# One load moved ahead of another in the start-up, and the elementwise work of the last layer (scaled halves of the token shift, low parts of the squares, splits of w_r and w_v) spread anew over ScalarE, VectorE and GpSimd

## The reference, cut to what matters

```python
x = attention(q, k, v, i_gate, f_gate, o_gate)     # (2, 768, 320)
# MoE1: gated layer that mixes over the tokens
h = relu(x @ w_in); u, v = h[..., :512], h[..., 512:]
v_n = (v - mean(v)) / sqrt(var(v) + 1e-6)
v_s = einsum('ts,bsd->btd', w_spatial, v_n) + b_spatial
y = (u * v_s) @ w_out                               # (2, 768, 320)
# MoE2: token shift, squared relu, sigmoid gate
y_prev = y shifted by one token (0 at the first)
xk = mu_k * y + (1 - mu_k) * y_prev
xr = mu_r * y + (1 - mu_r) * y_prev
k = relu(xk @ w_k)                                  # (2, 768, 1024)
out = sigmoid(xr @ w_r) * ((k * k) @ w_v)
```

## Time and profile before

| what | value |
|---|---|
| median of 3 runs | 332.5 us (332.32 to 332.51) |
| the profiled execution's own time | 331.42 us |
| its span in the trace | 329.70 us |
| TensorE busy | 311.5 us (94%) |
| VectorE busy | 213.9 us (65%) |
| ScalarE busy | 140.7 us (43%) |
| GpSimd busy | 69.2 us (21%) |
| mean granted TensorE clock | 0.978 of full |

### The profile page before, as it was taken

The page is one execution under the profiler, slowest core; times in us unless marked ns, Lnnn a source line. Parts: engine busy times, 40 slices in busy tenths (PEclk is TensorE's granted clock), DMA queues, the critical chain, the costliest instruction groups (busy, mean ns, idle before and its releaser), DMA issues.

```text
span 329.7 us, 5470 instructions
## 1 busy us (share of the span) xinstructions
PE 311.5 (94%) x1952; PEld 297.8 (90%) x1952; DVE 213.9 (65%) x458; ACT 140.7 (43%) x271; POOL 69.2 (21%) x94
## 2 busy tenths in 40 slices
PE   7899889999999999678999999999799999999996
PEld 3798789999999999579999999999699999999996
DVE  7788798767567747653642689979489536845111
ACT  4945574333332332550313354367584255336000
POOL 8622413012212100511111120214041013013000
PEclk9989879999999999999999999999799999999999
DMA  5994122022234207200006002040000100010011
GB/s 155 272 226 120 56 82 73 22 71 84 84 98 127 75 4 231 88 0 3 0 2 191 0 2 61 2 159 0 2 0 7 56 1 2 20 40 2 20 51 50
DMA packets 11374, 20.92 MB, mean 63 GB/s; under 512 B 1908, under 2 KB 5508, under 8 KB 11348
## 3 DMA queue, kind: packets, MB, share of 16 engines
q1 hardware_dynamic: 11348, 20.58, 21.1%
HBM read 18.53 MB, written 1.97 MB: 62 GB/s over the span
## 4 chain that ended last, share of the span: by engine, by line
PE 73%; DVE 14%; issue 4%; ACT 4%; DMA 3%; SPq 1%; POOL 1%; DVEq 0%; ACTq 0%; POOLq 0%
PE ps_v L1079 17%; PE ps_s L1079 10%; PE ps_e L1079 7%; PE ps_in L1079 6%; PE ps_out L1079 6%; PE ps_t L1079 6%; PE ps_in L1157 4%; PE ps_z L1079 4%; PE ps_s L1148 4%; DMA qkt<-in_qk 3%; PE ps_out L1167 2%; PE ps_z L1176 2%; DVE kr L1051 1%; PE ps_e L1125 1%; DVE pt L804 1%
## 5 line engine op out<-in xcount | busy, mean ns | idle before, releaser
L539 POOL TENSOR_TENSOR kkl<-kr,kkh 128x384 fp32r<-128x384 f32 x16 | 17.6, 1097 | 73.4 <-ACT kkh L694 73.4
L1051 DVE TENSOR_TENSOR kr<-kr 128x384 f32<-128x384 f32 x32 | 20.4, 641 | 14.5 <-ACT kr L737 14.5
L1148 PEld LDWEIGHTS ps_s<-qkt 128*128 128x128 f32 x192 | 25.9, 200 | 3.6 <-DMA qkt<-in_qk 2.0
L1148 PE MATMUL ps_s<-qkt 128*128 128x128 f32 x192 | 27.1, 287 | 1.7 <-DMA qkt<-in_qk 1.7
L1157 PEld LDWEIGHTS ps_in<-tok,pt 128*128 128x128 f32 x192 | 24.6, 195 | 0.9
L1157 PE MATMUL ps_in<-tok,pt 128*128 128x42 f32 x192 | 24.4, 278 | 0.0
L1079 PE MATMUL ps_v<-win,xth 128*128 128x512 f32 x60 | 21.9, 431 | 1.3 <-DVE xtl L885 1.3
L710 ACT ACTIVATE gh<-ut 128x384 fp32r<-128x384 f32 x16 | 8.4, 525 | 33.4 <-DVE ut L1016 33.3
L574 ACT ACTIVATE et<-ps_e 128x512 f32<-128x512 f32 x24 | 14.3, 595 | 18.8 <-PE ps_e L1130 14.4
L534 POOL TENSOR_TENSOR gl<-ut,gh 128x384 fp32r<-128x384 f32 x8 | 9.5, 1183 | 58.5 <-ACT gh L710 58.5
L1079 PE MATMUL ps_v<-xth,win 128*128 128x384 f32 x65 | 19.1, 359 | 2.5 <-ACT vr L580 1.4
(11 more groups left out here) (293 smaller groups left out, 917.1 us busy)
## 6 DMA issues: line engine op xcount, KB each, us to landing
tok<-in_vk SPq DMA_DIRECT2D x12, 328.0 KB, 4.3
qkt<-in_qk SPq DMA_DIRECT2D x24, 160.0 KB
sp_raw<-in_w_sp SPq DMA_DIRECT2D x6, 384.0 KB, 5.0
osig<-in_og SPq DMA_DIRECT2D x2, 960.0 KB, 10.5
out_y<-ob SPq DMA_DIRECT2D x12, 160.0 KB, 1.8
wv_raw<-in_w_v SPq DMA_DIRECT2D x2, 640.0 KB, 4.9
win_raw<-in_w_in SPq DMA_DIRECT2D x4, 256.0 KB, 7.0
wk_raw<-in_w_k SPq DMA_DIRECT2D x2, 512.0 KB, 4.5
```

Of the source, the lines that this page charges most:

```text
L539: gp.tensor_tensor(kkl[a % 2][:, b, :], kr[n % 4][:, :], bits(kkh[a % 2][:, b, :]), ALU.subtract).then_inc(sems["kk_lo_pool"], 1)
L1051: ve.tensor_tensor(kr[n % 4][:, :], kr[n % 4][:, :], kr[n % 4][:, :], ALU.mult).then_inc(sems["kk_done"], 1)
L1148: last = te.matmul(ps_s[j][:, h * CH:(h + 1) * CH], keys[u % NS][:, HH * j + h, :], queries[u % NS][:, h, :], start=True, stop=True)
```

## The change

It has five parts. (1) SyncE issues the features of the third chunk before the first half of w_in. (2) The `scaled` half of each shift step goes from VectorE to ScalarE: step 0 of a block behind the swap of y, step n+1 behind the same group as `shifted_hi` of step n, ahead of it. (3) All low parts of the squares are made on VectorE. (4) w_r is split earlier: ScalarE and VectorE behind sp(3,1), ScalarE behind sp(3,2), and the two full low blocks by GpSimd behind sp(3,2). (5) w_v is split by ScalarE behind k(0,3) to k(0,6), with a wait for its load, and by VectorE behind r(0,2) and the three groups of y(2). The load of w_v stays where it was.

```diff
+WV_LO = {("r", 0, 2): (0,), ("y", 2, TA): (1,), ("y", 2, TB): (2,), ("y", 2, TL): (3,)}
...
@@ SyncE
             load_tokens(1)
+            load_features(2)
             load_win(0)
-            load_features(2)
             load_win(1)
...
@@ GpSimd, in the loop over GROUPS
-                if kind == "k" and b % 2 == 0:
-                    n = 8 * a + b
-                    pool.wait_ge(sems["kk_hi_done"], n + 1)
-                    gp.tensor_tensor(kkl[a % 2][:, b, :], kr[n % 4][:, :], bits(kkh[a % 2][:, b, :]),
-                                     ALU.subtract).then_inc(sems["kk_lo_pool"], 1)
+                if key == ("sp", 3, 2):
+                    for t in range(2):
+                        pool.wait_ge(sems["wr_hi"], 2 + t)
+                        gp.tensor_tensor(wr[:, 2 + t, :], wr_raw[:, t, :], bits(wr[:, t, :]),
+                                         ALU.subtract).then_inc(sems["wr_lo"], 1)
...
@@ ScalarE
+            def scale(a, n):
+                t, w = n // 2, n % 2
+                i = 6 * a + n
+                if i == 0:
+                    act.wait_ge(sems["mu_in"], 16)
+                act.wait_ge(sems["y_copied"], 2 * a + 2)
+                if t == TL:
+                    act.wait_ge(sems["y_left"], a + 1)
+                if i > 1:
+                    act.wait_ge(sems["x_shifted"], i - 1)
+                sc.activation(scaled[:, n % 2, :], yt[a % 2][:, t, 1:NB + 1], ACT.Copy,
+                              scale=mucol[:, w, t:t + 1]).then_inc(sems["x_scaled"], 1)
...
+                    if (a, b) == (3, 1):
+                        left_hi(wr, wr_raw, "wr_in", 64, "wr_left", "wr_hi")
+                    if (a, b) == (3, 2):
+                        rows_hi(wr, wr_raw, "wr_left_lo", "wr_hi")
...
                     sc.activation(ysw[64:128, :], ps[0:64, 0:NB], ACT.Copy).then_inc(sems["y_swapped"], 1)
+                    scale(a, 0)
                 if kind == "k":
                     n = 8 * a + b
-                    if n == 0:
-                        left_hi(wr, wr_raw, "wr_in", 64, "wr_left", "wr_hi")
-                        rows_hi(wr, wr_raw, "wr_left_lo", "wr_hi")
                     act.wait_ge(sems["group_mm"], p + 1)
                     if n >= 4:
-                        act.wait_ge(sems["kk_lo_pool"], (n - 4) // 2 + 1)
-                        act.wait_ge(sems["kk_lo_dve"], (n - 4 + 1) // 2)
+                        act.wait_ge(sems["kk_lo_dve"], n - 3)
...
-                    if a == 1 and 1 <= b <= 4:
-                        f = 2 * (b - 1)
+                    if a == 0 and 3 <= b <= 6:
+                        f = 2 * (b - 3)
                         act.wait_ge(sems["wv_in"], 32)
+                        act.wait_ge(sems["g_lo_pool"], 2 * NBLK)
+                        act.wait_ge(sems["g_lo_dve"], 2 * NBLK)
                         sc.activation(wv_hi[:, f:f + 2, :], wv_raw[f // 4][:, f % 4:f % 4 + 2, :],
...
                 for i in SHIFTS.get(key, ()):
+                    if i % 6 < 5:
+                        scale(i // 6, i % 6 + 1)
                     shifted_hi(i // 6, i % 6)
...
@@ VectorE, shift()
-                if i > 1:
-                    dve.wait_ge(sems["x_shifted"], i - 1)
-                ve.tensor_scalar(scaled[:, n % 2, :], y[:, t, 1:NB + 1], mucol[:, w, t:t + 1], None,
-                                 ALU.mult).then_inc(sems["x_scaled"], 1)
                 dve.wait_ge(sems["x_scaled"], i + 1)
...
+                    if (a, b) == (3, 1):
+                        left_lo(wr, wr_raw, "wr_left", "wr_left_lo")
...
-                    if n == 0:
-                        left_lo(wr, wr_raw, "wr_left", "wr_left_lo")
-                        rows_lo(wr, wr_raw, "wr_hi", "wr_lo")
...
-                    if b in (2, 4, 6):
+                    if b > 0:
                         square_lo(n - 1)
                     if b == 7:
                         square_lo(n)
-                    if a == 1 and 2 <= b <= 5:
-                        f = 2 * (b - 2)
-                        dve.wait_ge(sems["wv_hi_done"], b - 1)
...
+                for i in WV_LO.get(key, ()):
+                    f = 2 * i
+                    dve.wait_ge(sems["wv_hi_done"], i + 1)
+                    ve.tensor_tensor(wv_lo[f // 4][:, f % 4:f % 4 + 2, :], wv_raw[f // 4][:, f % 4:f % 4 + 2, :],
+                                     bits(wv_hi[:, f:f + 2, :]), ALU.subtract).then_inc(sems["wv_lo_done"], 1)
...
@@ TensorE, before the first v group of a block
-                        pe.wait_ge(sems["kk_lo_pool"], 4 * a + 4)
-                        pe.wait_ge(sems["kk_lo_dve"], 4 * a + 4)
+                        pe.wait_ge(sems["kk_lo_dve"], 8 * a + 8)
```

More of the change, by code:

```diff
@@ L147 @@
 gate_m gate_next gates_in group_mm gwt_done head_rows_done ident_done ident_zero later_done later_zero ones_done k_relu
-kk_done kk_hi_done kk_lo_dve kk_lo_pool kw_done kw_zero mix_biased mix_gated mrow_in
+kk_done kk_hi_done kk_lo_dve kw_done kw_zero mix_biased mix_gated mrow_in
 mu_done mu_in nm_hi_done nm_zero nm_lo_done num_done o_in0 o_in1 osig_done out_done0 out_done1 out_ready
@@ L1056, in _ @@
                         square_lo(n)
-                    if a == 1 and 2 <= b <= 5:
-                        f = 2 * (b - 2)
-                        dve.wait_ge(sems["wv_hi_done"], b - 1)
-                        ve.tensor_tensor(wv_lo[f // 4][:, f % 4:f % 4 + 2, :], wv_raw[f // 4][:, f % 4:f % 4 + 2, :],
-                                         bits(wv_hi[:, f:f + 2, :]), ALU.subtract).then_inc(sems["wv_lo_done"], 1)
+                for i in WV_LO.get(key, ()):
[3 more added lines that the diff above has]
+                                     bits(wv_hi[:, f:f + 2, :]), ALU.subtract).then_inc(sems["wv_lo_done"], 1)
                 if kind == "v":
```

## The result

| | median | lowest to highest | runs |
|---|---|---|---|
| kernel before, run beside it | 332.5 us | 332.32 to 333.99 | 4 |
| changed kernel | 329.51 us | 327.85 to 330.02 | 4 |

The medians differ by 3.0 us; the forecast was 329.6. The ratio of the two kernels is 0.9892 (95% interval 0.9846 to 0.9938).

The account below looks back on a forecast made before the run. TensorE bounded the kernel, losing 4.17 us to its wait for VectorE at k(1,0) and the half clock behind it. Gains of 1.2 (wait) and 1.7 (clock), 2.9 together, took 332.5 to 329.6; range 328.0 to 332.0.

Parts of the forecast that it names:

- The sum: Whole kernel: 1.2 us less wait at k(1,0), 1.7 from the clock, 0 from the rest, 2.9 less in all.
- The path through w_v's load: ScalarE in k(0) waits 0.8 for w_v, step 11 completes at 232.0, the wait at k(1,0) shrinks from 2.49 to 1.3.
- the slower rival: w_v's load holds ScalarE and delays step 11 one for one; landing at 224 gives 333.9 us; chance 0.12.
- The table load: Before the first sigmoid: 1.28 by the trace; the skill's further drain of 1.38 would leave the wait at k(1,0) unshrunk.
- The scaled half on the path: Step 11's scaled copy on ScalarE, between first sigmoid and `shifted`: taken at 0.53 us, bounds 0.41 to 0.73.
- The clock: Behind k(1,0): a stall of 1.3 us keeps the full clock, another 1.7 gained; rival that it falls, chance 0.17.
- The prediction's second leg: TensorE's 2.0 us stall for `sp_lo` kept the clock at 1.00, so the shorter stall of 1.3 should too.
- Features first: Start-up: w_in's first half lands at about 21.2, harmless up to 21.8; value nothing, at worst a loss of 0.5 us.
- The first relu "because nothing stands between": Head of k(0): with w_r's pieces gone, the first relu comes at about 217.5 instead of 219.76.
- The load of w_v "where it was": End of sp(3): last product with u unmoved, so w_v's load is issued at 215.37 and lands at 221.4.
- The cause named: In sp(3,3), GpSimd's two low parts of w_r, 0.85 us each, can hold up VectorE, returning its saving on scaled halves.
- The squares' low parts: In k(0), moving them from GpSimd to VectorE is even for VectorE, from nothing to 0.5 us better.

Follow-up runs that it names:

- E8: Changed kernel with three more ScalarE copies, computing nothing new, ahead of the first sigmoid: median 332.93 us, ratio 1.0018.
- E3: Changed kernel with shift steps 10 and 11 behind k(0,0) and k(0,1) instead of r(0,0) and r(0,1): median 326.86 us, ratio 0.9878.
- E6: Changed kernel with the split of w_v put back in k(1): median 328.04 us, ratio 0.9873.
- E7: Changed kernel with the split of w_r put back at the head of k(0): median 327.9 us, ratio 0.9862.
- E5: Changed kernel with the scaled halves back on VectorE: median 335.09 us, ratio 1.0065.
- E9: Kernel before with only the scaled halves moved to ScalarE: median 326.75 us, ratio 0.9847.
- E1: Kernel before with only the third chunk's features issued ahead of w_in's first half: median 331.84 us, ratio 1.0013.
- E2: Changed kernel with w_in's first half issued ahead of the third chunk's features again: median 329.24 us, ratio 0.9933.
- E4: Changed kernel with the low parts of the even squares back on GpSimd: median 329.41 us, ratio 0.9937.
- E11: Kernel before with only the squares' low parts all made on VectorE: median 328.79 us, ratio 0.9888.
- E12: Changed kernel with w_r's two full low blocks moved from GpSimd in sp(3) to VectorE at the head of k(0): median 328.74 us, ratio 0.9892.
- E10: Kernel before with scaled halves on ScalarE and all the squares' low parts on VectorE: median 328.14 us, ratio 0.9878.

## Why the prediction was right, and where its terms were not

**The sum.** Predicted 2.9, made of 1.2 of wait and 1.7 of clock. Measured from S on 1.18 and 1.63, and 3.0 between the medians. That the median met the forecast to 0.1 is luck: the interval of the ratio is 0.46% wide to each side, 1.5 us, where the prediction had thought that 0.2% could be told. The two sections of the profile, 2.81 together, are the better witness.

**The path through w_v's load** is right. ScalarE's wait 1.00 (0.8 predicted), table load 17.05 behind S (17.24 predicted: 227.95 less 210.71), wait at k(1,0) 1.31 (1.3). From the first piece of w_v to the table load it was 6.55, as summed up. Behind the table load it was 4.30 and not 4.08, mostly since `shifted` began 0.29 behind the end of the scaled half (231.41 to 231.70) and not 0.03; the table load's being 0.19 sooner made up for it. E8 shows that nothing of the path is slack, E3 that all of the wait goes when step 11 leaves it, E6 and E7 that it goes, or shrinks to 0.37, when w_v's pieces leave ScalarE or the load comes in time. "One for one" with the landing, as the slower rival had it, was not tested by itself: in E5 the first relu was late too.

**The table load.** The sigmoid started 1.29 behind the start of the load again (229.17 to 230.46). The further drain of 1.38 that the Trainium skill counts (ScalarE: Activation LUTs, What ACT_TABLE_LOAD costs) isn't seen here either; by it, as an estimate, the wait would have been 2.7.

**The scaled half on the path** was taken at 0.53 and took 0.61, inside its bounds. Each of the 24 costs ScalarE more than VectorE, as the Trainium skill says of operations with a fast mode on VectorE (Perfetto Trace Analysis, Optimizing Scalar/DVE Operations), and the trace agrees (0.61 against 0.41). The page names a saturated VectorE as the case in which moving such work may make sense; it doesn't say "only", as the prediction has it. VectorE's 65% of the whole span would have misled here: up to the end of sp(3) VectorE was the engine that set the first relu and w_v's load, and E9, this part alone, gave the best ratio of all.

**The clock.** Kept, as predicted. Behind k(1,0), waits of 2.3 to 3.8 in the lists (before, E1, E5, E8) all dropped it, and waits of 0.2 to 1.1 (changed, E2, E4, E7, E11, E12) never did. Nothing between was measured there. The prediction's second leg, that a stall of 2.0 keeps it, was one execution's luck: see the end.

**Features first.** Nothing, as predicted: w_in's first half landed near 20.8 (21.2 in E1), predicted 21.2, under the 21.8 from which it would cost.

**Two terms were credited to the wrong part,** and their errors cancelled.

- *The first relu "because nothing stands between".* It did come 2.8 earlier (6.26 behind S for 9.05; predicted 217.5, 6.79). But not from w_r's pieces: without moving them it is 6.35 (E7) and 6.36 (E9). It comes from the scaled halves, for which the prediction had allowed 0.45 at step 9, with the rest given back to GpSimd's pieces. They save 2.69 there, 1.38 of it before sp(3) began, where the prediction had looked for nothing. w_r's pieces give 1.88 at the head of k(0) (from step 9's high part to the first relu 0.43, and 2.31 in E9) and take 1.78 in sp(3) (step 9's high part 5.83 behind S in the changed kernel, 4.05 in E9). E5 agrees: w_r moved without the scaled halves makes the first relu no sooner than before, but later (9.67 for 9.05).
- *The load of w_v "where it was".* It was, to 0.46 (4.20 for 4.66), because part 4 gave back 1.79 of the 2.24 that part 2 gained (E9: 2.42). E7 shows the price: 0.94 of wait. The cause named was GpSimd; E12 shows that it is VectorE's stand for ScalarE, and less than 0.1 of GpSimd.

**The squares' low parts,** "for VectorE this is even, from nothing to 0.5 better", turned out otherwise where nothing hides them: they shorten relu to table load by 1.16 (E11). The prediction had priced every collision by the one square of 1.10, which is 0.56 dearer than one of 0.54; two of the three that count cost 0.8. It had priced a low part at 0.55, and one behind the other they come every 0.47. In the changed kernel the prediction came out right all the same, since ScalarE's wait for w_v hides it (E4).

**What the whole could have been.** In steps, by the wait at k(1,0): before 2.49; part 2 takes it to 0 (E9), part 3 adds nothing (E10), parts 1 and 5 bring 0.37 (E7), part 4 another 0.94. Such a list depends on its order: part 3 alone takes the wait to 1.21 (E11). Part 2 alone gives 4.17 from S on against 2.81, and the best median, 326.75. The ratios agree in direction, but their intervals overlap (0.9823 to 0.9871 against 0.9846 to 0.9938), so that it beats the changed kernel is shown by the sections of the profiles, 1.36 us, more than by the medians.

## What to carry to other kernels

Price the parts of a change each by itself and against each other: here either of two parts (2 and 3) gave the gain alone, and two others (4 and 5) took back a third of what was to be had. Work that is moved ahead of the operation that releases a load delays the load, and a piece that waits for a load holds all that the engine's stream has behind it; look for both before "sooner" is booked as a gain. Where an engine's share is far below full, read the stretch in which it sets the next start: VectorE at 65% of the span was the bound of the stage that ends with sp(3).

## What the runs showed of the hardware that was not expected

**The start-up differs from execution to execution.** S lies between 210.10 and 214.94, though the kernels differ little up to there. The start of the second part, the first matmul behind TensorE's wait for `sp_lo`, lies between 148.59 (E3) and 151.88 (E6), in kernels that are alike up to there save for the order of two loads. From it to S it is 61.5 in eleven profiles and 63.05 to 63.07 in the three of the next paragraph (E5, E6, E8). So 3.3 of E6's 4.84 come from the start-up and 1.55 from the clock behind that wait. The clock is at 0.50 in different places of the first 60 us. The same window in E6 and E3:

```profile
16.00:30.00 14.00, 14.00 (x70) 13.61 (x68) 9.41 (x26) 7.04 (x15) 3.18 (x4) 0.51 0.75 199
```

```profile
16.00:30.00 14.00, 12.67 (x80) 12.37 (x81) 11.37 (x32) 7.68 (x17) 2.93 (x3) 0.76 0.61 180
```

E3 got through ten more matmuls in these 14 us at a mean clock of 0.76 than E6 at 0.51. The mean clock of the start-up doesn't tell the loss, though: over the first 60 us it is 0.91 in E2 (second part from 148.66) and in the changed kernel (150.59), and 0.97 in E8 (148.64). The number of matmuls done by then does: 342, 323 and 342, and 313 in E6. In the profiles these differences before S are the larger part of the spread; the runs of before spread as widely (of the 29 beside E1, 26 took 328.95 to 333.46 and three up to 335.62), more than the change itself, and some intervals here are 1% wide. What decides where the clock is low wasn't tried.

**The same stall, two outcomes.** TensorE waits 2.0 for `sp_lo` in all profiles. In eleven of the fourteen, that of before among them, it was followed by a clock of 1.00; in three (E5, E6, E8) by one of about 0.50, at a cost of 1.5 us. The end of the stall in E6, and a window of E5 just behind it:

```profile
151.88 0.41 PE L1096 MATMUL ps_e<-sp_hi,vnh 128*128 128x384 f32 x1 [2.01 <-DVE sp_lo L832]
```

```profile
152.00:153.00 1.00, 1.00 (x5) 1.00 (x4) 0.00 (x0) 0.00 (x0) 0.00 (x0) 0.50 0.00 0
```

So one trace with a stall that kept the clock doesn't say that a stall of this length keeps it.
